# Router lanes and counts moved onto VectorE and between its mask rows, a placement step one pair later, and two early gathers behind a pair's sums

## The reference

```python
scores = scale * q @ k.T; scores[causal] = -1e9
local = softmax(scores) @ v
q_p = phi(q)                       # elu(q) + 1
mem_out = (q_p @ M_prev) / (q_p @ z_prev + 1e-6)
x = g * mem_out + (1 - g) * local  # as [2304, 512], g = sigmoid(beta) for each head
logits = x @ w_gate
e_idx = argmax(logits)             # one expert of 8 for each token
gate_w = softmax(logits)[e_idx]; eom = sigmoid(x @ w_output_gate)[e_idx]
out = gate_w * eom * (relu(x @ w1[e_idx]) @ w2[e_idx])
```

## Time and profile before

| | |
|---|---|
| median of 3 runs | 464.05 us (464.01 to 465.46) |
| the profiled execution | 464.11 us, its span 462.2 us |
| busy share of the span | PE 98%, DVE 66%, ACT 60%, POOL 42% |
| granted TensorE clock | 0.998 |
| chain that ended last, by engine | PE 97% |
| the experts' part (209.56 to the end) | 252.64 us |

### The profile page before, as it was taken

One profiled execution on the slowest core, in us unless ns is written; L12 is line 12 of the kernel. 1 busy time (PEld: TensorE's weight loads), 2 busy tenths in 40 slices (PEclk: granted clock), 3 DMA queues, 4 the chain that ended last, 5 costly groups with the idle time before them and its releaser, 6 DMA issues.

```text
span 462.2 us, 11671 instructions
## 1 busy us (share of the span) xinstructions
PE 453.9 (98%) x4252; PEld 355.9 (77%) x4252; DVE 303.8 (66%) x780; ACT 276.9 (60%) x622; POOL 195.3 (42%) x192
## 2 busy tenths in 40 slices
PE   8999999999999999999999999999999999999995
PEld 6677777677777777787888888888888888888884
DVE  4889898989999997877222399222237957952220
ACT  5889988999999875344222577222237837832221
POOL 7567776769889846251222111221111312221111
PEclk9999999999999999999999999999999999999999
DMA  7234433567544723647322279410117966600000
GB/s 232 83 113 143 134 105 106 191 200 221 194 119 143 239 58 98 210 124 272 129 69 69 72 242 342 171 38 13 46 48 236 326 238 193 223 1 23 23 24 37
DMA packets 44883, 64.09 MB, mean 139 GB/s; under 512 B 7198, under 2 KB 26142, under 8 KB 44832
## 3 DMA queue, kind: packets, MB, share of 16 engines
q1 hardware_dynamic: 40672, 53.81, 35.2%
q0 software_dynamic: 4160, 9.60, 6.5%
HBM read 56.77 MB, written 10.90 MB: 146 GB/s over the span
## 4 chain that ended last, share of the span: by engine, by line
PE 97%; ACT 1%; issue 1%; DVE 0%; another core or an unknown queue 0%; POOL 0%; ACTq 0%; POOLq 0%; DVEq 0%
PE S L1469 23%; PE S L1652 19%; PE S L1653 18%; PE S L1654 18%; PE STK L1469 4%; PE TP_ps L1469 4%; PE TP_ps L1465 3%; PE TP_ps L1692 2%; PE STK L1465 2%; PE STK L1687 2%; PE S L1465 1%; ACT w_hi0b L778 0%; PE TP_ps L1675 0%; DVE probs L970 0%
## 5 line engine op out<-in xcount | busy, mean ns | idle before, releaser
L749 ACT ACTIVATE probs<-probs,neg_max 128x128 f32<-128x128 f32 (+2 forms) x144 | 82.8, 582 | 5.1 <-DVE neg_max L970 4.5
L695 POOL DMA_INDIRECT out<-x_ring,slot_tok_i x23 | 26.9, 1171 | 134.9 <-ACT x_ring L835 102.9
L1652 PE MATMUL S<-w_hi,x_hi 128*128 128x512 f32 x180 | 70.2, 390 | 0.0
L1654 PE MATMUL S<-w_hi,x_lo 128*128 128x512 f32 x180 | 70.1, 389 | 0.0
L1653 PE MATMUL S<-w_lo,x_hi 128*128 128x512 f32 x180 | 70.0, 389 | 0.0
L618 POOL DMA_INDIRECT x_ring<-x_tokens,slot_tok_i x29 | 32.0, 1105 | 85.2 <-DMA out<-x_ring,slot_tok_i 67.9
L1469 PE MATMUL S<-k_pair,q_pair 64*128 64x256 f32 (+5 forms) x384 | 64.3, 442 | 0.0
L1652 PE MATMUL S<-w_hi0b,hid_hi 128*128 128x512 f32 x152 | 61.7, 406 | 0.0
L970 DVE CUSTOM_DVE_ANT_0 probs<-S,mask 128x128 f32<-128x128 f32 (+3 forms) x128 | 55.1, 487 | 6.8 <-PE S L1469 6.3
L1653 PE MATMUL S<-w_lo0b,hid_hi 128*128 128x512 f32 x152 | 59.4, 391 | 0.0
L1654 PE MATMUL S<-w_hi0b,hid_lo 128*128 128x512 f32 x152 | 59.2, 389 | 0.0
(11 more groups left out here) (230 smaller groups left out, 875.9 us busy)
## 6 DMA issues: line engine op xcount, KB each, us to landing
w_raw<-in_moe_w SPq DMA_DIRECT2D x60, 512.0 KB, 5.3
q_pair<-in_qt SPq DMA_DIRECT2D x15, 288.0 KB, 2.9
k_pair<-in_kt SPq DMA_DIRECT2D x15, 288.0 KB, 3.4
v_nat<-in_v SPq DMA_DIRECT2D x16, 256.0 KB, 3.5
x_tokens<-x_out SPq DMA_DIRECT2D x16, 256.0 KB, 2.4
x_ring<-in_moe_w SPq DMA_DIRECT2D x2, 512.0 KB, 4.9
m_aug<-in_m_aug SPq DMA_DIRECT2D x1, 648.0 KB, 6.6
m_turned<-in_m_t SPq DMA_DIRECT2D x1, 512.0 KB, 3.6
```

Source lines behind the costliest of these rows:

```text
L695: nc.gpsimd.indirect_dma_start(out=out[:, :], out_offset=bass.IndirectOffsetOnAxis(ap=slot_tok_i[:, t:t + 1], axis=0), in_=x_ring[:, t % X ...
L749: last = nc.scalar.activation(pr, pr, ACT.Exp, bias=neg_max[:, slot, h:h + 1], scale=-1.0, accum_out=sums[g % 2][:, at, 0:1])
L1652: T.matmul(dst, hi, part(i, k)[:, cols], start=first, stop=False)
L1654: return T.matmul(dst, lo, part(i, k)[:, cols], start=False, stop=last)
```

## The change

- lanes(0) and lanes(1) leave GpSimd; VectorE does them, some in routing_ahead (pairs 9, 10, 11, 13), some in a new routing_between(g), which stands behind read_loc and ahead of the masks of slots 3 to 6 (pairs 13 and 15). The semaphore placed goes.
- so_far(1, 1) goes from routing_ahead(8) to routing_between(10); so_far(2, 3) from routing_behind(13) to routing_between(14).
- order_rest goes from pair 12 to pair 8; place(2) from routing_behind(14) to routing_ahead(15).
- GpSimd issues gather 0 where it issued all three; gathers 1 and 2 follow the sums of pair 14 (x == G - 2) in the next iteration.

```diff
@@ gpsimd
-            def lanes(b):
-                pool.wait_ge(r_consts_dve, 1)
-                pool.wait_ge(placed, b + 1)
-                for t in range(b * TPB, (b + 1) * TPB):
-                    nc.gpsimd.tensor_scalar(r_lanes[:, t, :], iota_f[:, :], r_lane[:, t:t + 1], None, ALU.is_equal).then_inc(lanes_done, 1)
...
                                             mem_x[u][:, :, :, 0:D], ALU.add).then_inc(x_added, 1)
+                    if x == G - 2:
+                        for t in range(1, EARLY_TILES):
+                            gather(t, gather_first[t], LAST * S)
...
-                elif 0 <= g - 9 - KD < 2:
-                    lanes(g - 9 - KD)
...
-                    for t in range(EARLY_TILES):
-                        gather(t, gather_first[t], LAST * S)
+                    gather(0, gather_first[0], LAST * S)
@@ vector
+            def routing_between(g):
+                if g == 10:
+                    so_far(1, 1)
+                elif g == 13:
+                    lanes(1, 0, 2)
+                elif g == 14:
+                    so_far(2, 3).then_inc(hot_done, 1)
+                elif g == 15:
+                    lanes(1, 4, 5)
...
                     turns()
-                    so_far(1, 1)
+                    order_rest()
                 elif g == 9:
                     place(0)
+                    lanes(0, 0, 2)
                 elif g == 10:
                     largest(1)
                     choose(1)
+                    lanes(0, 2, 3)
                 elif g == 11:
                     open_gate(1)
                     so_far(1, 2)
+                    lanes(0, 3, 5)
                 elif g == 12:
                     place(1)
-                    order_rest()
                 elif g == 13:
                     largest(2)
+                    lanes(1, 2, 4)
                 elif g == 14:
                     scale(0, LAST)
                 elif g == 15:
+                    place(2)
                     early_tiles()
                     lanes(2, 0, 3)
...
                 elif g == 13:
                     choose(2)
-                    so_far(2, 3).then_inc(hot_done, 1)
                     open_gate(2)
                 elif g == 14:
                     read_ranks(2)
-                    place(2)
...
                 if valid(x):
                     read_loc(x)
+                if valid(g):
+                    routing_between(g)
```

More of the change, by code:

```diff
@@ L277, in memory_attention_top1_moe @@
     scale_stored = [sem(f"scale_stored{n}") for n in range(2)]
-    placed = sem("placed")
     lanes_done = sem("lanes_done")
@@ L1132, in place @@
                 link(V.tensor_scalar(r_tile_of[:, ts, E], r_part[:, ts], ROUND, -ROUND, ALU.add, ALU.add))
[L1133 to L1137, removed]
+                link(V.scalar_tensor_tensor(r_lane[:, ts], r_tile_of[:, ts, E], -float(P), r_slot[:, ts], ALU.mult, ALU.add))
             def lanes(b, first=0, end=TPB):
```

## The result

Before and after were run in turn on one chip, six times each. Before took 463.81 us (463.19 to 465.46), after 467.80 us (466.93 to 470.41). The ratio is 1.0092, with a 95% interval of 1.0071 to 1.0114: 4.0 us slower, by medians. The forecast was 467.6 us.

What follows compares the result with a forecast made beforehand. TensorE was taken to bound the kernel, waiting one to one for VectorE's fourth-slot mask. Terms 0.85 + 0.66 + 0.54 + 0.68 + 0.84 gave + 3.57 on 464.05, 467.6 us; range 463.1 to 468.8.

Steps and rivals of the forecast that it cites:

- The bound and the model: TensorE waits one to one for VectorE's fourth-slot mask; a pair is mask start + 2.06 + the rest.
- The signs of being wrong: Wrong if lanes beside phi_T take 0.28, products trail the mask under 2.06, or ScalarE's last copy follows early tokens sooner.
- pairs 9 and 10: Before pair 10's fourth mask: two lanes 0.40, so_far(1, 1) 0.35, hold of its cast 0.10; + 0.85 us.
- pair 13: Two lanes before the fourth mask, held by phi_T and the logits' sum: mask at + 2.10, + 0.66 us.
- pair 14: Cast of so_far(2, 3) held by phi_T, mask at + 1.60; place(2) leaves; + 0.54 us.
- pair 15, lane and place(2): Held lane ahead of the fourth mask + 0.68, then place(2) ahead of the early tiles + 0.84 us.
- gathers: Gathers 1 and 2 behind pair 14's sums on GpSimd: price 0, last issue at 179.0 latest, 0.5 us kept.
- free-lanes rival: GpSimd lets VectorE's small operations through in phi_T: + 0.58 us, 464.6 us; chance 0.25.
- order_rest: Moved to pair 8: 0 either way; its absence in pair 12 shortens nothing that TensorE waits for.
- place(2): In pair 15 ahead of the early tiles: + 0.84 us, with no VectorE idle time to hide it.
- early-landing rival: No hold, and gather 0 alone lands sooner, saving up to 1.66 us: 463.0 us, down to 462.3; chance 0.18.
- Whole lock: q_pos holds to its end, pair 10's fourth mask 0.65 later, pair 11's second lane up to 0.4: 468.4; chance 0.10.

Runs made afterwards that it cites:

- probe: Before plus one unused 128-column operation ahead of the fourth slot's mask in pairs 4 to 7: profiled 466.15 us with tensor_scalar, 463.77 us with tensor_reduce.
- gathers only: Before with only the gathers' order changed (gather 0 alone, gathers 1 and 2 behind pair 14's sums): 463.16 us against 463.28, ratio 0.9999.
- count-back experiment: After with so_far(1, 1) back in pair 8, so only the lanes are new in pairs 9 and 10: 467.85 us, ratio 1.0087.
- q_pos first: Before with after's gathers' order, order_rest in pair 8 and GpSimd's lanes behind q_pos instead of ahead: 463.18 us against 463.79, ratio 0.9997.
- place(2) back: After with place(2) back behind pair 14's last mask, as in before: 466.50 us, ratio 1.0062.
- cleared kernel: After with nothing between read_loc and the fourth slot's mask, the same operations placed elsewhere on VectorE: 466.62 us, ratio 1.0077.
- both together: After with nothing between read_loc and the fourth slot's mask, and place(2) behind pair 14's last mask: 465.09 us, ratio 1.0025.

## Why the prediction was right, point by point

**The bound and the model.** Right. In pair 13 the fourth mask starts at the pair's start + 2.04 (142.78 to 144.82) and in the probe the pairs grew one to one with the mask. Mask start + 2.06 + the rest gave 11.70, 11.58 for pairs 13 and 14; the trace has 11.60 (142.78 to 154.38) and 11.46 (154.38 to 165.84). The value products follow the mask by 2.03 in pair 14, which leaves a rest of 7.93 where 7.92 stood.

**The signs of being wrong.** Two of the three came up by the letter, and neither was one. The products follow by 0.03 less than 2.06, which is too little to take TensorE's wait away. And ScalarE's copy of the last pair came sooner after the early tokens, 3.94 us instead of 5.61:

```profile
180.47 0.22 ACT L758 ACTIVATE out_T<-S 128x64 f32<-128x64 f32 x1
```

But it comes after 3.95 us in before, run again, with all three gathers together. The mask of pair 10, forecast at its pair's start + 1.1, came at about + 1.55 (110.71 to 112.26), which is the miss below.

**The sum**, forecast and measured, in us:

| term | forecast | measured | how read |
|---|---|---|---|
| pairs 9 and 10 | + 0.85 | + 1.45 | shift of pair 13's start against before (142.78 and 140.32), net of pair 1's mask |
| pair 13 | + 0.66 | + 0.56 | 11.60 less 11.04 |
| pair 14 | + 0.54 | + 0.42 | 11.46 less 11.04 |
| pair 15, lane and place(2) | + 1.52 | + 1.29 | start of pair 15 to slot_tok_i: 10.69 (165.84 to 176.53) less 9.40 |
| gathers | 0 | 0 | gathers only: 155.44 and 5.57 |
| sum | + 3.57 | + 3.72 | |

The nearness of the two sums is in part luck: pairs 9 and 10 cost 0.60 more than forecast, and the other terms together 0.45 less.

**Pairs 9 and 10: the term that was mis-sized**, by 0.60, and by 0.64 at pair 10's own mask, which came 1.49 later. I priced the lanes at 0.40, from a row where GpSimd does nothing, and kept the hold by q_pos for a rival in which q_pos holds from first to last. Neither is what happened. r_tile_of (106.73, 0.60 long) and r_lane (107.36, 0.17) passed inside q_pos, as in before; the lanes behind them did not, and both ended with it. A free middle and a held end is a case that I had not put up, although the trace of before had it: the cast of the earlier trace rows that took 0.506 started at 149.00, 1.17 behind q_pos's start, and ended with it (149.48). The count-back experiment gives 0.88 for the lanes, 0.48 over my 0.40. The cast was priced at 0.10 of hold, and the count as a whole at 0.45; it took 0.62. VectorE was by then later than I had placed it, and met not phi_T's end (111.59) but the logits' sum that starts at 111.79. So the count was placed in time without the delay of the lanes ahead of it, and met GpSimd's work at the wrong part; the lanes were placed rightly and priced without their hold.

**Pairs 13, 14 and 15: held lanes and casts**, right within 0.26 together (1.62 against 1.88, place(2) apart) and in mechanism. The lanes of pair 13 ended with phi_T and with the sum, as forecast (+ 2.10 forecast, + 2.04 measured); masks of pairs 14 and 15 at + 1.50 and + 1.56 where + 1.60 stood. The probe shows that such a lane costs by its hold and not by its work: 0.85 us a pair against 0.00. The free-lanes rival is out. Its condition, lanes of 0.28 us beside phi_T, was met nowhere.

**order_rest**: I had written that its absence in pair 12 shortens nothing that TensorE waits for. The version with q_pos first has pair 13's mask 0.14 sooner by it, and my own sum had that in, where VectorE comes to pair 13's mask at + 0.40.

**place(2)**: 0.84 in the rows (172.37 to 173.21), but the stretch from pair 15's mask to slot_tok_i grew by only 0.65 (9.13 against 8.48 in before). The cover is a short wait that I had not seen: from the three lanes' start to the eighth mask it is 0.76 in before (168.71 to 169.47) and 0.59 in after (173.62 to 174.21), so before's mask waited 0.17 there. I had written that VectorE has no idle time here. This term is plain work on the path; no hold is in it.

**The gathers**: right in the price of 0, not in the place. The last gather was to go out at 179.0 at the latest, with the whole kernel's shift at slot_tok_i (4.73) at 183.7. It went out at 185.11, since GpSimd's sums ahead of it took 2.0 us longer than elsewhere (the third point of the last section). Still nobody waited: TensorE's turn of tile 1 comes 13.25 us behind slot_tok_i (189.78), as in before, run again (13.26). The bound of 0.5 wasn't needed. The early-landing rival had read one execution's chance wait as a transfer: in the kernel before, run again, it is absent, and with the gathers' order alone the time is 0.9999 of before. I had noted what spoke against it and still gave it 0.18.

**Whole lock**: it gave 468.4, and the measured 467.8 lies between it and the forecast. It was right on the place that I missed: it put pair 10's mask 0.65 later than my sum, and it came 0.64 later. As a whole it is wrong, since two operations passed inside q_pos ahead of the lanes; and the 0.4 that it put on pair 11 did not come, as the two lanes there (128.93) took 0.48 together, which is their free length. The Trainium skill (SBUF — State Buffer, section Who interferes with whom) has the shared pair locked for the whole instruction; phi_T's rows agree (a lane of 1.32 us ended with it); of q_pos's rows the lanes of pair 9 agree, and r_tile_of, r_lane and the lanes of pair 11 don't.

**The time.** 463.8 + 3.72 is 467.5, against a median of 467.8. In the profiled execution the start was 1.0 us later than in before's, and before's had 0.8 us of chance wait; the two nearly cancel, which is why the spans (466.2 and 462.2) differ by what the medians do.

## What to carry to other kernels

Before an operation moves to VectorE, look which operation of GpSimd is running at its new place, after all delays ahead of it are added: 0.28 us of work beside a two-input sum cost 0.85 us a time here, and a reduce of the same length nothing, both in a place with 0.29 us to spare. Where nothing is to spare, add the work itself. A small operation that is cheap in the table of groups may be so only where it stands; of its price at the new place, a probe in four pairs tells more than its mean. And a gap that one trace shows before a copy is to be seen in a second execution before a forecast is built on it.

## What the runs showed of the hardware

- GpSimd's one-input operation over 576 columns (q_pos, 1.66 us) and its two-input one (phi_T, 1.41 us) hold VectorE differently. Beside phi_T every lane waited to its end, in the traces of after, the probe, place(2) back and the count back. Beside q_pos it is the moment that decides for a lane, not its kind or size: two lanes that started 0.65 us behind its start took 0.28 each (after, 128.93), two that started 0.93 behind it waited to its end (after, 107.56), and so did a cast 1.17 behind it (before, 149.00). What starts at once is held for a part only: r_tile_of ended 0.70 us behind q_pos's start, and in the cleared kernel a cast beside q_exp (the same kind and size as q_pos) 0.68 behind that one's. The end does not hold everything: r_hot, of two inputs, 1.22 behind q_pos's start (before, 116.13), took its usual 0.20. Why the middle is free is open. So the two engines meet not only at semaphores.
- Beside phi_T the hold goes by the kind of operation: tensor_scalar 1.32 us, tensor_reduce 0.28 us, same columns read and same place. Size doesn't free it: a tensor_scalar over 5 columns was held too, beside low_ahead.
- It goes the other way too. In after, GpSimd's last sums met VectorE's two-input splitting of weights: logits_h took 1.53 us (179.60) and x_out 2.53 us (181.10), where x_out takes 1.56 elsewhere. Nobody waited for them.
- The granted clock fell to 0.50 for about 3 us in both traces of the cleared kernel, behind 0.99 us of idle TensorE, and cost 1.6 to 1.7 us: 7.17 and 7.28 instead of 5.58 from slot_tok_i to the last turn. In after and in the count back, with the same 0.99 us, it did not fall. It fell for about 3 us near the start as well, between the masks of pairs 0 and 1, in three of the twelve traces: before again (0.50 from 12 to 14 us), place(2) back and both together (0.50 from 14 to 16 us). The cause is open.
- That fall near the start is some 2 of the 3 us by which the two latest starts (19.43 and 19.45) stand apart. From pair 0's fourth mask to pair 1's it is 8.74 or 8.75 us in the nine traces without it, 10.71 and 10.67 in place(2) back and both together, and 10.04 in before again. Of the last combination's ten timed runs the four at 467.8 us have a mean clock of 0.994, the six at 464.1 to 465.2 one of 0.997 or more; and the run of after at 470.41 has 0.995, its other five 0.998 or more. Where the clock doesn't fall, pair 1's mask starts at 15.5 to 17.4 us. The landing of the first input is a part of that: TensorE's first scores start at 3.57 us in before and, after a wait for that transfer, at 4.12 in after.
